# Turning the first head's probabilities ahead of the second head's scores, with the normalisation between the two masks

## The reference

```python
scores = scale * np.matmul(q, k.transpose(0, 1, 3, 2))
thresh = np.max(scores, axis=-1, keepdims=True) - tau
scores = np.where(scores >= thresh, scores, -1000000000.0)
scores = scores - np.max(scores, axis=-1, keepdims=True)
attn = np.exp(scores)
attn = attn / (np.sum(attn, axis=-1, keepdims=True) + 1e-09)
return np.matmul(attn, v).astype(np.float32)
```

## Time and profile before

| | us |
|---|---|
| median of 3 runs | 1072.77 |
| lowest and highest run | 1070.63, 1074.0 |
| time of the profiled execution | 1073.18 |
| its span | 1071.5 |
| mean granted TensorE clock, share of full | 0.985 |

### The profile page before, as it was taken

One profiled execution on the slowest core, in us unless ns is written; L12 is line 12 of the kernel. 1 busy time (PEld: TensorE's weight loads), 2 busy tenths in 40 slices (PEclk: granted clock), 3 DMA queues, 4 the chain that ended last, 5 costly groups with the idle time before them and its releaser, 6 DMA issues.

```text
span 1071.5 us, 19367 instructions
## 1 busy us (share of the span) xinstructions
PE 1031.0 (96%) x6519; PEld 899.5 (84%) x6520; DVE 538.2 (50%) x1205; ACT 388.8 (36%) x812; POOL 336.7 (31%) x443
## 2 busy tenths in 40 slices
PE   6999999999999789999999998999999999999997
PEld 5888888888888668888888887989999999999996
DVE  5687887888888601222111214654444444434442
ACT  4567666667666222322232322322111111211111
POOL 2133335312112398699957272001010010100101
PEclk9899999999999889999999999999999999999999
DMA  6465677657644365546554345100000000000000
GB/s 170 104 162 133 156 184 191 166 149 196 145 105 129 117 220 183 176 160 205 198 172 158 119 150 158 68 1 30 30 30 30 1 29 29 29 0 0 30 1 30
DMA packets 103504, 116.38 MB, mean 109 GB/s; under 512 B 70269, under 2 KB 70301, under 8 KB 102917
## 3 DMA queue, kind: packets, MB, share of 16 engines
q1 hardware_dynamic: 88228, 87.51, 29.7%
q10 hardware_dynamic: 11056, 13.69, 4.0%
q0 software_dynamic: 4144, 14.20, 3.7%
HBM read 68.53 MB, written 18.82 MB: 82 GB/s over the span
## 4 chain that ended last, share of the span: by engine, by line
PE 81%; DVE 5%; ACT 4%; DMA 4%; issue 3%; SPq 2%; POOL 0%; DVEq 0%; POOLq 0%; ACTq 0%
PE bank L682 73%; PE bank L685 8%; ACT exps L1052 3%; DMA k_st<-k_both 3%; DVE probs L1287 1%; DVE neg_max L1276 1%; SPq L435 1%; SPq L446 1%; DVE X L1319 1%; DMA x_sorted<-X,pos 0%; DMA x_row<-x_sorted 0%; DMA qraw<-in_q 0%; DVE ring L1577 0%; ACT q_hi L1068 0%; DVE q_lo L1305 0%
## 5 line engine op out<-in xcount | busy, mean ns | idle before, releaser
L682 PE MATMUL bank<-x_hi,ring 128*128 128x384 f32 x768 | 210.8, 337 | 0.5 <-DVE act L1635 0.5
L682 PE MATMUL bank<-ring,g_hi 128*128 128x512 f32 x576 | 179.1, 392 | 0.0
L1218 ACT ACTIVATE g_hi<-act 128x384 fp32r<-128x384 f32 x96 | 50.4, 525 | 302.6 <-DVE act L1635 300.1
L585 POOL TENSOR_TENSOR ring<-stage,ring 128x2048 fp32r<-128x2048 f32 x32 | 147.1, 4597 | 4.8
L1052 ACT ACTIVATE exps<-bank,neg_max 128x576 f32<-128x576 f32 x144 | 106.8, 742 | 103.0 <-DVE neg_max L1276 62.6
L682 PEld LDWEIGHTS bank<-x_hi,ring 128*128 128x128 f32 x768 | 140.3, 188 | 4.3 <-DVE act L1635 0.9
L682 PE MATMUL bank<-k_st,q_st 128*128 128x288 f32 (+5 forms) x696 | 128.4, 321 | 11.3 <-DVE probs L1287 8.9
L1276 DVE TENSOR_REDUCE neg_max<-bank 128x1 f32<-128x576 f32 x144 | 109.1, 758 | 48.4 <-PE bank L682 42.7
L1632 DVE TENSOR_SCALAR neg<-bank,alpha_col 128x384 f32<-128x384 f32 x96 | 59.1, 616 | 144.0 <-PE bank L682 144.0
L682 PE MATMUL bank<-x_lo,ring 128*128 128x384 f32 x384 | 128.9, 336 | 0.0
L682 PEld LDWEIGHTS bank<-ring,g_hi 128*128 128x128 f32 x576 | 106.8, 188 | 18.7 <-DVE g_lo L1583 0.3
(11 more groups left out here) (181 smaller groups left out, 1432.6 us busy)
## 6 DMA issues: line engine op xcount, KB each, us to landing
stage<-in_moe_w SPq DMA_DIRECT2D x32, 1024.0 KB, 5.4
k_st<-k_both SPq DMA_DIRECT2D x60, 288.0 KB
x_row<-x_sorted ACTq DMA_DIRECT2D x23, 296.0 KB, 2.9
y_sorted<-y_row ACTq DMA_DIRECT2D x21, 256.5 KB, 2.9
q_st<-q_hi SPq DMA_DIRECT2D x30, 160.0 KB
q_st<-q_lo SPq DMA_DIRECT2D x30, 160.0 KB
qraw<-in_q SPq DMA_DIRECT2D x16, 256.0 KB, 3.3
vraw<-in_v SPq DMA_DIRECT2D x16, 256.0 KB, 4.8
```

What stands on the lines that cost most here:

```text
L585: nc.gpsimd.tensor_tensor(lo, src, hi.bitcast(F32), ALU.subtract).then_inc(piece_lo, 2)
L682: return nc.tensor.matmul(dst, lhsT, rhs, start=start, stop=stop)
L1218: nc.scalar.activation(g_hi[f % 3][:, :], act2[f % 2][:, :], ACT.Copy).then_inc(g_hi_ready, 1)
```

## The change

PE: `turn_probs` of head 0 moves up, ahead of `turn_out` and of the second head's scores. ACT: the second head's exponentials no longer wait for the normalisation. DVE: the splits now come directly behind the maxima, then the mask of head 0, then a wait for the second head's exponentials, then the routing step (three units) and the normalisation, then the mask of head 1. In a pair's last unit, which has one tile, the order is maximum, split, normalisation, mask. Nothing is added to or taken from the arithmetic or the DMAs.

```diff
@@ PE, pair
                     if more:
                         scores(*nxt, 0)
+                    turn_probs(n, j, 0)
                     if not (static(n) and j < 3):
                         turn_out(*((n, j - 3) if j >= 3 else (n - 1, j + UNITS - 3)))
                     if more and nxt[3] < MAIN:
                         scores(*nxt, 1)
-                    turn_probs(n, j, 0)
                     if j < MAIN:
                         turn_probs(n, j, 1)
@@ ACT, exp_tile
-                if h == 1 and UNITS * n + j >= 4:
-                    act.wait_ge(x_ready, UNITS * n + j - 3)
@@ DVE, pair
                     for h in heads_of(j):
                         maxima(n, j, h)
-                    for g in range(3):
-                        if (n, j) == route_unit(g, 8):
-                            route_step(g, 7)
-                    if not (static(n) and j < 4):
-                        normalise(*((n, j - 4) if j >= 4 else (n - 1, j + UNITS - 4)))
                     if (n, j) == (0, 0):
                         scale_emb()
                     if (n, j) == (0, 2):
                         place_params()
                     if job:
                         split(job[0], job[0] % 2, job[1])
-                    for h in heads_of(j):
-                        mask(n, j, h)
+                    if j < MAIN:
+                        mask(n, j, 0)
+                        dve.wait_ge(exp_done, tile_no(n, j, 1) + 1)
+                    for g in range(3):
+                        if (n, j) == route_unit(g, 8):
+                            route_step(g, 7)
+                    if not (static(n) and j < 4):
+                        normalise(*((n, j - 4) if j >= 4 else (n - 1, j + UNITS - 4)))
+                    mask(n, j, heads_of(j)[-1])
                     if not (static(n) and j == 0):
                         inverse(*before(n, j))
```

## The result

The kernel with the change took **1077.39 us** in the median of 11 runs (1074.54 to 1081.13), the kernel before, run beside it, 1071.49 (11 runs). The ratio is 1.0062, 95% interval 1.0042 to 1.0081: slower by about 6.6 us (the two medians lie 5.9 apart). The profiled execution took 1076.66 with a span of 1075.0, against 1073.18 and 1071.5, so this pair of traces is only 3.5 apart. Its mean granted clock is 0.990 (0.985 before). In the profile after, some lines have moved by two: the mask's instruction is L1285, the exponentials L1050, the maximum L1274, `q_hi` L1066, the normalisation L1317.

The account below looks back on a forecast made before the run. It took the loop through DVE to bound units without a split, PE most of the rest, late queries some seams. Seams +3.1, unit gains -1.1, PE's starts +0.3, threshold +0.5: +2.8, so 1075.6 us, range 1067 to 1082.

Parts of the forecast that it names:

- The step that failed: First pair: nothing to normalise yet, the same nine turns ahead of the next first mask, so cost 0.
- The sum at the seams: Between pairs, behind late query DMAs: waits cost 2.65 us before and 5.8 after, so +3.1.
- the wait w: ScalarE's wait for late query DMAs at a seam: costs w - 1.02 before, about w - 0.50 after.
- no change: Rival, chance 0.17: DMAs starting 0.2 sooner land sooner by more, or elsewhere; only the small gain is left, 1072.
- Unit without split: Unit 2 of every pair and nearly all units of the last two: second exponentials no longer wait, gain 0.10, 3.85 us.
- Units with split: Units 0 and 1 of a pair: DVE is busy from maximum to last mask in any order, gain 0.
- At a seam that PE bounds: Between pairs where PE is the bound: moved turns leave once and come in once, 0.
- The fit: Units 0, 1 and 2: moved turns fit into PE's wait before `turn_out` to within 0.01, cost 0.
- The threshold: Normalisation behind a mask waiting for POOL's threshold adds 0.2 to each such unit, +0.5 in all.
- PE's gaps fill: Rival, chance 0.18: loop shorter than read, PE becomes the bound, about -12, 1061; decides if maximum-to-second-mask falls under 1.75.
- Slower by a held first mask: Rival, chance 0.22: first mask held by threshold or turns, +8, with seams 1084; or PE late at `turn_out`, +4.

Follow-up runs that it names:

- seam_old: Changed kernel with the turns of a pair's last unit put back behind the next pair's second scores: 1071.98 us, ratio 1.0017 to the kernel before.
- pe_alone: Kernel before with the turns of head 0 moved up on PE alone, VectorE and ScalarE as before: 1083.29 us, ratio 1.0115.
- dve_alone: Kernel before with VectorE's and ScalarE's edits alone, PE as before: 1071.94 us, ratio 1.0007.
- best: Changed kernel, turns moved up only in units 0 to 3 outside the first pair, last unit's normalisation ahead of the split, two DMA semaphores: 1058.49 us, ratio 0.9890.
- pair0_old: Changed kernel with the turns of head 0 back behind both scores in the first pair alone: 1071.08 us, ratio 1.0016 to the kernel before.
- before_pair0_new: Kernel before with the turns of head 0 moved up in the first pair alone, nothing else of the change: 1075.95 us, ratio 1.0042.
- both_old: Changed kernel with the turns of head 0 back behind both scores in the first pair and every pair's last unit: 1068.65 us, ratio 0.9984 to the kernel before.
- both_norm: Changed kernel, turns moved up only in units 0 to 3 outside the first pair, last unit's normalisation ahead of the split: 1064.65 us, ratio 0.9947 to the kernel before.

## Why the prediction was right, and where it was wrong

Forecast 1075.6 (1067 to 1082), measured 1077.39; by the profiled executions +2.8 forecast and +3.5 measured. That the total is near is luck in good part. The kernel before, run beside it, was at 1071.49 and not at the 1072.77 on which the forecast was built, so the change costs 5.9 to 6.6 us, about twice the forecast's +2.8. In the profiled executions, 1.5 us of the kernel before are its lower clock at 650.9 us. And one term of the sum was wrong by more than its whole result.

**The step that failed** is the one that cost the first pair at nothing: "In the first pair there is nothing to normalise yet, and the same nine turns stand ahead of the next first mask: 0." The same turns do stand there, but not the same scores. I counted instructions and did not look at the form: only in the first pair the scores are 64-row matmuls, and the loss is in what they share when nothing stands between the heads. Measured in its place: 1.19 in one unit (6.20 against 5.01) and in the next (6.34 against 5.15), and there are three such units, so about 3.6, an estimate; 2.76 in S10 of the profiled execution; 0.42% or 4.5 us when done alone, with an interval of 2.7 to 6.4. Neither the list of rows nor a bound covered it; every row of the forecast was of 60 us and later.

**The sum at the seams was right, its form was not.** 2.65 was forecast before and 2.24 measured, 5.8 and 5.77 after, so +3.1 forecast and +3.5 measured. The form was another: I kept the wait w and raised its price from w - 1.02 to w - 0.50. In the trace the price stayed (1.72 for a wait of 2.67, so w - 0.95), and the waits grew, 1.83 to 2.67 in the same pair. PE comes to the seam 0.44 sooner, and the DMAs do not: the same loss told from the other side. It can be read from the end of VectorE's last split, which lets the DMAs go. In the pair of the longest wait the high part of the queries starts 11.86 behind it in the kernel before (260.94 to 272.80) and 12.20 in the kernel after (265.29 to 277.50). Less the waits, ScalarE was ready after 10.03 and 9.53. So 0.50 of that wait's growth is ScalarE being ready sooner, and 0.34 the DMAs landing later in that pair. In the seven seams whose wait in the kernel before was 0.76 or more, ScalarE is ready after 10.02 to 10.05 before and 9.52 to 9.63 after, while the DMAs let it start after 11.36 before and 11.41 after, in the mean. All seven waits grew, so "DMAs that start 0.2 sooner land sooner", on which *no change* rested, did not happen.

`seam_old`, which keeps the 0.44, is ready after 9.5 and has the long waits (16.5 us, 13 times). `pe_alone`, whose other units are longer, is ready after 10.2 and has short ones (8.2 us). `dve_alone` is in between, ready after 9.8, yet its list has only 9.4 us, 10 times: the landings vary from trace to trace by some tenths.

**Unit without split:** forecast 3.85, measured 3.81, and by pairs 0.15 instead of 0.10. It stood in all 13 pairs, 1.95, where I counted it in six and in the last ones only. **Units with split:** 0 forecast, 4.03 measured one way, and 20.61 less 20.46 leaves nothing for them. **At a seam that PE bounds** the turns leave at one end and come in at the other, 0: so it was, 0.44 each way, as an undisturbed pair of `seam_old` shows (20.02 instead of 20.46). What I didn't see is that the second could be had without the first. **The fit** of the turns into the wait: `turn_out` waits for nobody and is not late. That the fit has two sides is shown by `pe_alone`: without the early first mask it costs 0.42 a pair.

**The threshold** was put at +0.5, for normalisations behind waiting masks. It is one pair, whose POOL issues the DMAs for `x_sorted` just ahead of two thresholds, and 0.86 there. Behind the first pair all terms together are 3.53 - 1.95 + 0.86 = 2.44, measured 2.42.

**The end** gives some back. The kernel after is 5.18 us late at the fourteenth start of ten score matmuls (338.26 against 333.08), 4.72 at the fifteenth, as that pair is 0.46 shorter, and 3.5 at the end of the span. The last step lies in code that the change doesn't touch: 1.5 us come back in the stretch of lower clock at 650.9 us, some 0.3 go the other way.

**The rivals.** *No change* falls by the waits, which became longer and not shorter. *PE's gaps fill*, 1061, falls: maximum to second mask is 1.80, above its 1.75, and a pair won 0.15. By the Trainium skill (Perfetto Trace Analysis, Identifying the Most-Contended Engine) a weight-load share of 87% left room; the share after is 17.80 of 20.47, again 87%, while moving the turns gained 0.15. The room is there, since `best` takes 20.02, but what opened it was the order at the seam, not the share. *Slower by a held first mask* decides at 0.8 between second maximum and first mask; it is 78.20 - 77.52 = 0.68 in the ordinary unit and, of the units without a split, longer only in POOL's one pair, so that part of it falls, and PE is not late at `turn_out`.

**What stays open.** The first pair's loss is larger in the medians (4.5 and, from `pair0_old`, 4.9 us) and in S10 (5.2 between the means) than the 3.6 of the three units. The granted clock has a share in S10. The kernel before, in three stretches, in the columns of the earlier trace rows and then granted clock, DMA share and GB/s:

```profile
16.00:24.00 8.00, 6.61 (x31) 5.93 (x33) 6.02 (x15) 3.20 (x8) 0.77 (x4) 1.00 0.67 235
34.00:39.00 5.00, 5.00 (x33) 4.35 (x32) 2.40 (x6) 2.41 (x4) 0.57 (x3) 0.50 0.65 137
44.00:54.00 10.00, 9.61 (x82) 8.44 (x82) 8.57 (x21) 6.68 (x16) 3.35 (x11) 1.00 0.18 43
```

And nine turns in the second of them:

```profile
34.85 2.18 PE L685 MATMUL bank<-ident,probs 128*128 128x128 f32 x9
```

At a granted clock of 0.50, the lower of the two levels (1.2 GHz), nine turns last 2.18. Later, at 1.00 (2.4 GHz), they last 1.15. At 19.84 us they last 2.18 too, so PE ran at the lower level there, although the row from 16 to 24 us reads 1.00. That is inferred from the pace; no row of the first 20 us shows a lower clock, in any kernel.

The clock rises for good at a time that differs from kernel to kernel: at 40.0 us in the kernel before, 42.7 in the kernel after, 45.2 in `before_pair0_new` (whose S10 is the latest), 35.9 in `best` and 35.7 in `both_old` (the two earliest). From there to S10 it is 19.4 to 21.1 us in all of them. Three kernels without a turn between the first pair's scores (`best`, `both_old`, `pair0_old`) had a stretch at the higher level from 22 us on; no kernel with one had such a stretch before 31. With one trace a kernel, that may be the order of the turns or chance; no run tells. The 1.19 is free of it: in both kernels the first two such units run at the lower pace throughout (nine turns in 2.0 to 2.3).

The intervals of the kernel after and of `pair0_old` overlap a little (1.0042 and 1.0046), so the size of the first pair's loss is uncertain; its direction isn't, by `before_pair0_new`. Open too is why `both_norm` gained more than the pairs show.

## What to carry to other kernels

Cost a move in every form that the code takes: where the first round works with other tile shapes, look at rows of that round, and ask what stands back to back there. Where a chain is set free at one end and a DMA holds the other, the gain turns into a longer wait; give each consumer its own semaphore before an order is tuned. Where a wait is put down to one engine, look at which of the awaited semaphores really came last: the list named the threshold for 27 waits that were the turns'. And try a change in order at each place alone: here the same move gained in the middle of a pair and lost in the first pair and at the seam.

## What the runs showed of the hardware that was not expected

- Fifteen score matmuls of 64 rows, six and nine for the two heads, take 3.04 us back to back and 4.03 when four full-height turns stand between; one turn suffices (4.04). Back to back, the two heads' matmuls run in the same 0.65 us (17.54 to 18.19). The loads keep their length (324 ns) and overlap less. All this is at the lower pace; at the higher one, back to back, the fifteen take 2.00 (`best`, 22.75 to 24.75). The 128-row scores of later pairs take 0.61 to 0.63 per head in either order, at the higher clock, so the two forms aren't compared at one clock here.
- For 22 to 45 us from the start, by kernel, turns run at the pace of a granted clock of 0.50 (nine in 2.18 at 19.84, and 2.18 at 34.85, where 34 to 39 us reads 0.50), while the rows of that time read 1.00 in part. The pace of a known instruction tells the level where the row doesn't.
